# Who splits w_in, when tile 3's last scores are taken, and how the first keys land, in a one-core attention and MoE kernel

## The reference

```python
def _attn_ref(q, k, v, n_sink, window):          # 2 batches, 8 heads, 768 positions, head_dim 64
    scores = scale * np.matmul(q, k.transpose(0, 1, 3, 2))
    keep = is_sink | in_window                   # 4 sink positions, or the last 128 positions
    scores = np.where(keep, scores, -1000000000.0)
    a = np.exp(scores - np.max(scores, axis=-1, keepdims=True))
    a = a / (np.sum(a, axis=-1, keepdims=True) + 1e-09)
    return np.matmul(a, v)
def _moe_ref(x, w_in, w_out, g_ln):              # 1536 tokens, 512 -> 1024 -> 512
    h = x @ w_in
    e = np.exp(h - np.max(h, axis=-1, keepdims=True))
    solu = h * (e / (np.sum(e, axis=-1, keepdims=True) + 1e-09))
    ln = (solu - mean(solu)) / np.sqrt(var(solu) + 1e-06) * g_ln
    return ln @ w_out
def _moe2_ref(x, w_in, w_out):                   # 512 -> 2048 -> 512
    r = np.maximum(x @ w_in, 0.0)
    return (r * r) @ w_out
```

## Time and profile before

| | before |
|---|---|
| median of 3 runs | 505.79 us |
| the profiled execution | 507.02 us |
| its span, first to last instruction | 505.3 us |
| PE busy | 489.4 us (97%) |
| DVE busy | 277.7 us (55%) |
| ACT busy | 213.6 us (42%) |
| POOL busy | 101.6 us (20%) |

### The profile page before, as it was taken

How to read it: one execution, slowest core, us unless ns; L and a number is a source line. 1 busy time by engine, 2 the same in 40 slices (tenths; PEclk the granted TensorE clock), 3 DMA queues, 4 the chain that set the end, 5 groups by cost and what they waited for, 6 DMA issues and landing times.

```text
span 505.3 us, 7210 instructions
## 1 busy us (share of the span) xinstructions
PE 489.4 (97%) x2676; PEld 398.1 (79%) x2676; DVE 277.7 (55%) x499; ACT 213.6 (42%) x557; POOL 101.6 (20%) x139
## 2 busy tenths in 40 slices
PE   7979989999999999999999999999999999999997
PEld 5657768888788888878877888888888888888885
DVE  3889787788778778766597343342232233232222
ACT  4667456665656665634452332331221232121121
POOL 4645040220022022072995000000000000000000
PEclk9999989999999999999999999999999999999999
DMA  8931314323021110008000000020000002000002
GB/s 217 290 89 43 107 42 140 113 75 115 22 65 42 51 36 19 4 1 311 23 0 0 2 0 1 0 83 0 0 0 0 0 0 84 0 1 0 1 0 84
DMA packets 12837, 26.04 MB, mean 52 GB/s; under 512 B 1608, under 2 KB 2632, under 8 KB 12296
## 3 DMA queue, kind: packets, MB, share of 16 engines
q1 hardware_dynamic: 12504, 25.39, 16.2%
q10 hardware_dynamic: 304, 0.27, 0.2%
HBM read 22.51 MB, written 3.15 MB: 51 GB/s over the span
## 4 chain that ended last, share of the span: by engine, by line
PE 88%; DVE 6%; DMA 2%; SPq 1%; ACT 1%; issue 1%; POOL 1%; DVEq 0%; ACTq 0%
PE score_ps L1395 25%; PE h_ps L1407 12%; PE h_ps L1195 12%; PE w_ps L1233 12%; PE wt_ps L1407 6%; PE w_ps L1407 6%; PE o_ps L1165 4%; PE score_ps L1136 2%; PE wt_ps L1143 2%; DMA w2in<-w_in 2%; PE wt_ps L1136 1%; PE o_ps L1182 1%; PE h_ps L1223 1%; PE o_ps L1261 1%; PE w_ps L1251 1%
## 5 line engine op out<-in xcount | busy, mean ns | idle before, releaser
L1395 PE MATMUL score_ps<-x2T_hi,w2in_hi 128*128 (+1 forms) x192 | 74.9, 390 | 0.0
L1395 PE MATMUL score_ps<-x2T_hi,w2in_lo 128*128 (+1 forms) x192 | 74.7, 389 | 0.0
L1395 PE MATMUL score_ps<-x2T_lo,w2in_hi 128*128 (+1 forms) x192 | 74.7, 389 | 0.0
L1073 DVE TENSOR_TENSOR e<-e 128x512 f32<-128x512 f32 x24 | 18.5, 771 | 81.7 <-ACT e L772 81.7
L1073 DVE TENSOR_TENSOR sq<-relu 128x512 f32<-128x512 f32 x24 | 17.5, 728 | 80.2 <-ACT relu L772 80.2
L772 ACT ACTIVATE relu<-score_ps 128x512 f32<-128x512 f32 x24 | 14.3, 598 | 92.1 <-PE score_ps L1395 92.1
L772 ACT ACTIVATE e<-score_ps 128x512 f32<-128x512 f32 x24 | 14.4, 599 | 87.4 <-PE score_ps L1395 87.3
L1395 PEld LDWEIGHTS score_ps<-x2T_hi,w2in_lo 128*128 128x128 f32 x192 | 36.1, 188 | 7.5
L1395 PEld LDWEIGHTS score_ps<-x2T_lo,w2in_hi 128*128 128x128 f32 x192 | 36.0, 188 | 7.4
L1395 PEld LDWEIGHTS score_ps<-x2T_hi,w2in_hi 128*128 128x128 f32 x192 | 36.0, 188 | 7.4
L583 ACT ACTIVATE prob<-sm,nbias 128x132 f32<-128x132 f32 (+1 forms) x96 | 37.8, 395 | 0.5
(11 more groups left out here) (179 smaller groups left out, 1132.6 us busy)
## 6 DMA issues: line engine op xcount, KB each, us to landing
w2in<-w_in SPq DMA_DIRECT2D x4, 1024.0 KB, 4.8
w2out<-w_out SPq DMA_DIRECT2D x8, 512.0 KB, 7.2
V<-v SPq DMA_DIRECT2D x12, 256.0 KB, 2.7
k_raw<-kT SPq DMA_DIRECT2D x20, 132.0 KB, 2.8
q_raw<-qT SPq DMA_DIRECT2D x20, 128.0 KB, 2.8
w2in<-w_in SPq DMA_DIRECT2D x4, 512.0 KB, 7.8
w2in<-w_out SPq DMA_DIRECT2D x2, 1024.0 KB, 13.5
out<-u SPq DMA_DIRECT2D x6, 256.0 KB, 2.0
```

Source lines behind the costliest of these rows:

```text
L1073: nc.vector.tensor_tensor(sq[f % 2], relu[f % 2], relu[f % 2], ALU.mult).then_inc(sq_ready, 1)
L1395: done = mm(h2_ps[f % 2], ws[:, c, fs], xs[:, c, bass.ts(blk, BLK)], start=(c == 0 and i == 0), stop=(c == MC - 1 and i == 2))
```

## The change

Six edits, all in the lists up to the start of the regular steps.

1. DVE, not ACT, rounds chunk 0, right behind tile 0's second row_max; ACT starts with tile 0's bias and exponentials.
2. DVE splits chunks 0, 1 and 3, POOL only chunk 2, in four quarters of 256 columns. DVE's rounding of chunk 2 goes from ahead of tile 1's first merge to behind its second. ACT rounds chunk 3 behind four of tile 1's exponentials instead of ahead of all. On PE the products with chunk 3's high part go behind those with the low parts of chunks 0 and 1, and the first transposes of tile 1's probabilities go ahead of the products with chunk 3's low part.
3. DVE's `split_v_sink(0)` goes from tile 1's softmax to behind the split of tile 2's keys; tile 2's query split goes from DVE to POOL, behind POOL's last mask of tile 1. POOL rounds tile 2's keys before its queries.
4. The keys of tiles 0 and 1 land in two arrays of whole rows, sinks included (2112 bytes a row for four heads, where before each head's 528 or 512 bytes were a piece). Tile 1's score is two products, over 132 and 128 columns, 8 matmuls more in all.
5. In `first_step` the first transposes of tile 2's probabilities come after 5 of 8 high-part pairs of project_0 rather than after all, and DVE takes one split of w_out from second_step (into `split_w_out(2, 3)` at first_step's end).
6. In `second_step` on PE one matmul of project_0's low parts goes ahead of hidden(2), and tile 3's scores of pairs 2 and 3 go from behind transpose_ln(1) to between products 20 and 21 of hidden(2). ACT's `round_lnT(1)` goes behind all four first exponentials of tile 3, DVE's split_lnT behind tile 3's second row_max.

The core of the diff:

```diff
--- before.py
+++ after.py
...
@@ -339,11 +339,9 @@
                              ).then_inc(wo_loaded[c], 16)
 
             def load_k01(n):
-                src = slice(0, KS) if n == 0 else slice(N_SINK, KS)
-                dst = slice(0, KS) if n == 0 else slice(KS, W)
                 for half in range(2):
                     rows, heads = half_heads(half)
-                    sp.dma_start(k01[rows, :, dst], kT[n, :, heads, src]).then_inc(k01_loaded[n], 16)
+                    sp.dma_start(k01[rows, n, :, :], kT[n, :, heads, :]).then_inc(k01_loaded[n], 16)
 
             def load_v_sink(b):
                 sp.dma_start(v_sink_raw[0:SKS, b, :],
...
@@ -502,22 +501,22 @@
                                         ).then_inc(wo_split_pool, 1)
 
             def split_w_in(c):
-                pool.wait_ge(*((w_rounded, 2) if c == 2 else (w_rounded_act, c // 3 + 1)))
-                for half in range(2):
-                    cols = slice(half * BANK, (half + 1) * BANK)
+                pool.wait_ge(w_rounded, 3)
+                for part in range(4):
+                    cols = slice(part * F1 // 4, (part + 1) * F1 // 4)
                     nc.gpsimd.tensor_tensor(w_lo[:, c, cols], w_raw[:, c, cols], w_hi[:, c, cols].bitcast(F32),
                                             ALU.subtract).then_inc(w_split_pool, 1)
 
-            split_w_in(0)
+            split_w_in(2)
             build_v_sink(0)
             round_v_sink(0)
-            split_w_in(2)
-            split_w_in(3)
+            round_k(2)
             round_q(2)
-            round_k(2)
             halves(1, 0)
             gather_sinks(1)
             halves(1, 1)
+            nc.gpsimd.tensor_tensor(QL[0][:, :, :], q_raw[:, :, :], QH[0][:, :, :].bitcast(F32), ALU.subtract
+                                    ).then_inc(q_split, 1)
             for t in range(NT - 1):
                 inverse_std(t)
                 if t == 0:
@@ -702,11 +701,11 @@
                 bias(3, 0)
                 softmax_exp(3, 0)
                 softmax_exp(3, 1)
-                round_lnT(1)
                 copy_earlier(3, 2)
                 copy_earlier(3, 3)
                 softmax_exp(3, 2)
                 softmax_exp(3, 3)
+                round_lnT(1)
                 finish(1)
 
             def round_w_in(c):
@@ -718,7 +717,6 @@
                 nc.scalar.activation(KH[:, :, KEYS_SINKS[1]], raw_keys(1), ACT.Copy).then_inc(k_hi, 1)
 
 
-            round_w_in(0)
             bias(0, 0)
             for h in range(HG):
                 softmax_exp(0, h)
@@ -732,12 +730,14 @@
             round_xT(0)
             copy_earlier(1, 1)
             copy_earlier(1, 2)
+            copy_earlier(1, 3)
+            bias(1, 0)
+            for h in range(HG):
+                softmax_exp(1, h)
             round_w_in(3)
-            copy_earlier(1, 3)
-            for g in range(GROUPS):
-                bias(1, g)
-                for h in range(g * HG, (g + 1) * HG):
-                    softmax_exp(1, h)
+            bias(1, 1)
+            for h in range(HG, H):
+                softmax_exp(1, h)
             copy_pT(1, 0)
             copy_pT(1, 1)
             hidden_exp(0)
...
@@ -987,16 +988,16 @@
                 stats(1, 1)
                 variance(1)
                 split_xT(2)
-                split_w_out(2, len(WO_DVE))
+                split_w_out(3, len(WO_DVE))
                 normalize_hidden(1)
                 merge(3, 0)
                 merge(3, 1)
                 row_max(3, 0)
-                for part in range(2):
-                    split_lnT(1, part)
                 merge(3, 2)
                 merge(3, 3)
                 row_max(3, 1)
+                for part in range(2):
+                    split_lnT(1, part)
                 normalize_p(3, 0)
                 split_k(4)
                 split_q(4)
...
@@ -1019,27 +1020,29 @@
             row_max(0, 0)
             merge(0, 3)
             row_max(0, 1)
+            round_w_in(0)
             normalize_p(0, 0)
             round_w_in(1)
             normalize_p(0, 1)
-            round_w_in(2)
+            split_w_in(0)
             split_w_in(1)
             merge(1, 0)
             split_xT(0)
             merge(1, 1)
+            round_w_in(2)
             merge(1, 2)
             row_max(1, 0)
-            split_v_sink(0)
             merge(1, 3)
             row_max(1, 1)
             split_k(1)
             normalize_p(1, 0)
+            split_w_in(3)
             normalize_p(1, 1)
             hidden_max(0, 0)
             hidden_max(0, 1)
             hidden_max_all(0)
             split_k(2)
-            split_q(2)
+            split_v_sink(0)
             first_step()
             second_step()
             for t in range(EARLY, NT - 2):
...
@@ -1203,9 +1210,9 @@
                     pe.wait_ge(xT_rounded, 1)
                     pe.wait_ge(xT_split, 1)
                 if with_low:
-                    pe.wait_ge(*((w_split, 1) if c == 1 else (w_split_pool, 2 * max(c, 1))))
+                    pe.wait_ge(*((w_split_pool, 4) if c == 2 else (w_split, min(c + 1, 3))))
                 else:
-                    pe.wait_ge(*((w_rounded, c) if c in (1, 2) else (w_rounded_act, c // 3 + 1)))
+                    pe.wait_ge(*((w_rounded, c + 1) if c < 3 else (w_rounded_act, 1)))
                 for xs, ws in (((xT_hi, w_lo),) if with_low else ((xT_hi, w_hi), (xT_lo, w_hi))):
                     for half in range(2):
                         cols = slice(half * BANK, (half + 1) * BANK)
...
@@ -1327,15 +1335,17 @@
                 sink_values(2)
                 score(3, 0)
                 score(3, 1)
+                project_0(True, 2, 3)
                 pe.wait_ge(u_ready, 3)
                 hidden(2, 0, 12)
                 pe.wait_ge(u_ready, 4)
                 hidden(2, 12, 16)
-                project_0(True, 2, C1)
-                hidden(2, 16, 24)
-                transpose_ln(1)
+                project_0(True, 3, C1)
+                hidden(2, 16, 20)
                 score(3, 2)
                 score(3, 3)
+                hidden(2, 20, 24)
+                transpose_ln(1)
                 project(1, 0, 16)
                 transpose_p(3, 0)
                 transpose_x2(0)
@@ -1364,12 +1374,12 @@
             score(1, 3)
             hidden_0(1, False)
             hidden_0(2, False)
-            hidden_0(3, False)
             hidden_0(0, True)
             hidden_0(1, True)
+            hidden_0(3, False)
             hidden_0(2, True)
+            transpose_p(1, 0)
             hidden_0(3, True)
-            transpose_p(1, 0)
             keep_warm(1)
             transpose_p(1, 1)
             keep_warm(2)
```

33 lines of the change are left out of this document (20 added, 13 removed).

## The result

| | before | changed |
|---|---|---|
| median (range, runs) | 505.97 us (505.51 to 506.64, 6) | 503.72 us (503.11 to 504.15, 6) |
| ratio, 95% interval | | 0.9953, 0.994 to 0.9966 |
| profiled execution, span | 507.02, 505.3 | 503.94, 502.1 |
| PE, DVE, POOL busy | 489.4, 277.7, 101.6 | 489.4, 279.6, 99.0 |

The change saves 2.25 us here. 4.7 were forecast, and 503.72 lies just outside the range. The same kernel, timed again beside other groups of experiments, gave ratios of 0.998 (0.9963 to 0.9997) and 0.9966 (0.9948 to 0.9984): over the three the gain is 0.9 to 2.3 us.

A forecast was written before the change was run, and what follows sets the result against it. Up to 35.21 us the chain softmax, normalization, transposes was taken to set the pace, not PE's work. The head's -3.6 and second_step's -1.1 gave -4.7, from 505.8 to 501.1 us, range 499.2 to 503.6.

The forecast's parts named there:

- tile 0's softmax, to its transposes: Head, tile 0: bias 1.09 us sooner and z_eps 0.72 shorter, so transposes come at 11.1 instead of 12.92.
- transposes to hidden(1): Head, tile 1's first transposes to its hidden products: split of chunk 3 hidden, query split cost 0, bound +0.9.
- first_step, second_step: Steps after the head: first_step 0.1; second_step -1.1 us (bounds -0.3 and -1.9), with PE's long wait cut in two.
- hidden(1) starts later than 33: Sign of a wrong forecast: tile 1's hidden products, expected near 31.6 us, start after 33.
- Rival A: Only the head pays: the clock falls in second_step and PE loses 1.34 us again; 502.1 us, chance 0.15.
- the split is hidden, with a margin of 0.4: DVE's split of chunk 3 between tile 1's normalizations costs nothing, as POOL wants the second half's probabilities only later.
- Rival B: DVE is the head's new bound, still blocked by POOL; hidden starts 2.0 us earlier; 502.9 us, chance 0.13.
- the gain from POOL's blocking: Tile 1's merge to transposes: of up to 2.2 us DVE waits for POOL, 0.7 gained (bounds 0 and 1.9).
- whole rows at 0: Keys landing in whole rows may arrive 0.9 us sooner a tile, but gain 0 (bounds 0 and -0.3).
- the distance of 1.2 between profile and median: The median was put 1.2 us below the profiled execution's 507.0, giving 505.8 as starting point.
- Rival C: The head doesn't move: something taken for covered keeps tile 1's hidden products at 35.2; about 505.3 us, chance 0.08.
- D: Rival: slower, since the clock falls in the head in gaps around chunk 3; 506.8 us or more, chance 0.06.

The follow-up runs named there:

- before_again: The unchanged kernel before, run once more for a second profile; 28.77 us from first row_max to hidden(1), 469.72 from there to the end.
- keys_only: The kernel before with only the keys landing in whole rows; 505.20 us, ratio 0.9986.
- head_only: The changed kernel with first_step and second_step as before on PE, ACT and DVE; 505.06 us, ratio 0.9978.
- edit1_only: The kernel before with only chunk 0's rounding moved from ACT to DVE; 507.20 us against 506.58, ratio 1.0014.
- vsink_first: The changed kernel with POOL's product and cast of the sinks' values ahead of its quarters of chunk 2; 503.87 us, ratio 0.9942.
- q_late_vsink_first: The changed kernel with old key pieces, POOL's cast of tile 2's queries behind tile 1's masks, sinks' values ahead of chunk 2; 503.22 us, ratio 0.9941.
- round3_early: The changed kernel with ACT's rounding of chunk 3 put back ahead of tile 1's last copy of scores; 505.18 us, ratio 0.9969.
- second_only: The kernel before with only the second_step edit, all w_out splits left in second_step; 507.02 us, ratio 1.0007.
- pool_chunk1: The changed kernel with POOL splitting chunk 1, sinks' values loaded and prepared earlier, ACT rounding chunk 3 earlier; 505.45 us, ratio 0.9976.

## Why the prediction was wrong by half

The sum of -4.7 splits against the two profiles (505.3 to 502.1, -3.2) so:

| step | forecast | measured |
|---|---|---|
| start of tile 0 (first row_max) | 0 | 7.32 to 7.78, +0.46 |
| tile 0's softmax, to its transposes | -1.81 | 5.60 to 3.81, -1.79 |
| to tile 1's first merge | -0.7 | 4.73 to 3.90, -0.83 |
| merge to first transposes | -1.1 | 9.45 to 8.70, -0.75 |
| transposes to hidden(1) | 0 | 8.11 to 8.98, +0.87 |
| first_step, second_step | -1.1 | 470.09 to 468.93, -1.16 |

One of the prediction's own signs of being wrong came: hidden(1) starts later than 33, at 33.17.

**Right.** Tile 0: z_eps takes 0.17, the bias no longer waits. Second_step came as worked out: a new wait of 1.11 at the projection (1.2 forecast), 0.45 before tile 3's last transposes (0.55), then a wait of 0.74 for DVE's normalized values, which bound as expected, and a clock at 1.00:

The last view is a window of PE (busy us, count, granted clock, DMA share, GB/s):

```profile
69.00:74.00 5.00, 4.23 (x54) 1.00 0.44 146
```

Rival A's clock fall did not come. Against the executions with the old steps in which the clock doesn't fall there (before_again, keys_only and head_only, 469.65 to 469.80) the steps are worth 0.7 to 0.9 (edit1_only, at 470.11 without a fall there, loses 0.4 more ahead of hidden(2)); the 1.16 of the table is that and 0.4 of luck with the first profile.

**Wrong: what DVE does beside tile 1's last masks, taken as nothing.** This is the largest error in the head. The prediction put the stretch from the transposes to hidden(1) at 0; it was +0.87. It had read that POOL's last mask ends 5.3 behind the first transposes and hidden starts 2.8 later. The second half held (2.81). The first became 6.17: the last two masks began 4.04 behind the first transposes instead of 3.97, and then took 1.09 and 0.97 instead of 0.63 and 0.64, beside DVE's key split of tile 2 and the sinks' split. Edit 3 moved the sinks' split there, and the prediction took its 1.0 off tile 1's softmax and charged nothing at its new place. Its bound of +0.9 in this stretch was for the query split, which cost nothing: tile 2's scores followed the values without a wait. No run took these two operations away from the masks, so the cause is read from the rows; in vsink_first and q_late_vsink_first, where they meet one of the two last masks (1.14) and not the other (0.63 and 0.64), the stretch is 8.20.

**Used up, but nearly right: "the split is hidden, with a margin of 0.4".** The second transposes followed 2.70 behind the first, not 2.3, since the split took 1.63 and the product behind it 0.82: POOL's cast of the queries lay over the split, a mask over the product. The prediction left out what POOL's casts do to DVE there. But POOL's second pair of masks started only 0.07 later for it than before. What it hid is that POOL was ready 0.39 sooner (its wait at 28.23). Rival B came closest, 502.9, with transposes 2.9 and hidden 2.0 sooner, as measured. That is in part luck: it has the split of chunk 3 push the masks by 0.9, where they were pushed by 0.07 and lengthened by 0.79, and it has no late start of tile 0.

**Wrong in size: the gain from POOL's blocking.** Of the 2.2 us I let 0.7 be gained, 0.35 were. "POOL's multiplication for the sinks' values falls on the keys' split" stood in the text and was not given its price; it is 0.87 on KL and 0.40 on z_eps. What the halves of chunk 0 and 3 no longer blocked, the sinks' values and casts did. The experiments that moved single pieces of DVE's or POOL's work gained 0 to 0.4 up to hidden(1) in their profiles, for two reasons that the rows show: the blocking found a new place, and a second chain, ACT's rounding of chunk 3 and PE's products behind it, ends together with DVE's, so that a shorter DVE chain waits there (1.1 in both kernels with the sinks' values first). By the Trainium skill ("SBUF — State Buffer", "Who interferes with whom") a POOL operation that reads SBUF holds the shared ports for its whole length against a DVE operation with two SBUF inputs, and a `tensor_scalar` or cast in a two-port mode takes them too; the trace agrees for the one-input rounding of w_in (0.69 alone, 1.76 beside POOL's halves), while the merges that read PSUM stay at 0.44.

**Wrong: whole rows at 0.** I had looked for who waits for the keys, and for 0 or a gain. I had not asked what the faster queue does to the other one. Tile 0's queries landed 0.3 to 1.8 later, and PE waited for them in five of nine profiles; the price is 0.5 to 0.7. In the old order whole rows cost nothing that shows (keys_only 0.9986, an interval that still holds 1). There ACT and DVE wait for w_in; whether that comes sooner with whole rows isn't shown: ACT's first rounding stood at 8.00 in keys_only and at 7.83 to 9.20 in four profiles with the old keys. The page "DMA: Bandwidth & Descriptors" of the Trainium skill ("Queues, rings and completion order") has each DMA engine take turns between queues packet by packet. Larger rows on one queue would then cost the other its share; the landings agree, no run here looked at packets.

**Wrong: the distance of 1.2 between profile and median.** I subtracted it from the sum. But it was that one execution's, 0.4 of it a clock fall that the others with the old steps don't have; the profiled execution of the changed kernel lies 0.2 above its median. This is 1.0 of the 2.6 us by which the forecast missed; the head is the other 1.6 (-3.6 forecast, -2.04 measured): 0.87 at the masks, 0.46 at the start, 0.35 at the blocking, less 0.1 elsewhere.

Rival C is excluded (hidden(1) moved), and so is D as a forecast of this kernel, which is faster and has its clock at 1.00 through the head in all three profiles. But a fall of the clock in the head does occur in a near variant, round3_early.

Left open: whether the head of before, whose distance from row_max to hidden varies from 26.2 to 28.8 with the landing of w_in's chunks and with the clock, is on average 2.1 longer than the changed one's 25.4, as five profiles suggest (1.6 by the three of them without a clock fall in the head: before_again had one behind a wait of 3.15, second_only behind one of 2.70); where pool_chunk1 loses its 0.4 behind hidden(1); and what the sinks' values first give together with an earlier rounding of chunk 3.

## What to carry to other kernels

When work is moved away from an engine that blocks another, list everything that engine still does in that stretch, lay it over the other's operations one by one, and price each overlap; what is left over often finds a new place to block, and an operation that is moved has a price where it goes as well as a gain where it leaves. Then look which other chain ends at the same instruction: if it ends within 0.1 us of the one that you shorten, you gain nothing until both move. A transfer that nobody waits for still has a price if a faster form of it crowds out the transfer that the first instruction waits for. And take the difference between a profile and the median as part of the unknown, not as a constant: read a second execution's profile where one is to be had. Two variants of a kernel, too, can differ by 1 us only because one profile is of a slow execution and the other of a fast one.

## What the hardware showed that I had not expected

- The same wait doesn't always cost the same. The wait of 1.85 to 1.90 us before tile 3's last transposes was followed by a granted clock of 0.50 in one of five profiles (before) and by 1.00 in four (before_again, keys_only, head_only, edit1_only). Shorter waits were followed by 0.50 too: 1.15 in second_only, and waits of 1.03, 0.89 and 0.18 one after the other in round3_early.
- After the first row_max the changed order is steady: 25.38 to 25.41 us to hidden(1) in six profiles of it or of its head; the changed kernel's second profile had 25.85, with slower products on PE ahead of tile 0's transposes at a clock of 1.00. The row_max itself stood anywhere from 7.2 to 9.7.
- A POOL cast with one input blocks DVE as a two-input subtraction does (z_eps 0.57, split 1.63), and DVE blocks POOL's masks in turn (1.09 for 0.63, 0.97 for 0.64).
